# SyncE loads the next expert's first weights ahead of its x and the third unit later; GpSimd places two pooled steps between the last sums of v

## What is computed

```python
out_d = sm_attn(q_d, k_d, v_d)            # q_d, k_d, v_d: means over 4 positions (144 of 576)
out_up = np.repeat(out_d, factor, axis=2)
mask = np.abs(pos[:, None] - pos[None, :]) < factor
scores = np.where(mask, scale * np.matmul(q, k.transpose(0, 1, 3, 2)), -1000000000.0)
...
x = out_up + np.matmul(attn, v)
...
expert_idx = np.argmax(x @ w_gate, axis=1)
h = np.maximum(np.einsum('ecd,edf->ecf', disp, w1), 0.0)   # disp: the tokens of each expert
y = np.einsum('ecf,efd->ecd', h, w2)
...
h = x @ w_in
g = h * np.tanh(np.log1p(np.exp(h)))
return g @ w_out
```

## Time and profile before

| | before |
|---|---|
| median of 3 runs | 476.28 us (473.52 to 480.75) |
| the profiled execution | 477.65 us, span of its trace 475.5 us |
| TensorE busy | 447.9 us, 94% of the span |
| VectorE, ScalarE, GpSimd busy | 280.7, 230.1, 137.2 us |
| share of TensorE in the chain that ended last | 84% |
| moved by DMA | 74.97 MB, mean 158 GB/s |

### The profile page before, as it was taken

One profiled execution on the slowest core, in us unless ns is written; L12 is line 12 of the kernel. 1 busy time (PEld: TensorE's weight loads), 2 busy tenths in 40 slices (PEclk: granted clock), 3 DMA queues, 4 the chain that ended last, 5 costly groups with the idle time before them and its releaser, 6 DMA issues.

```text
span 475.5 us, 10038 instructions
## 1 busy us (share of the span) xinstructions
PE 447.9 (94%) x3380; PEld 412.8 (87%) x3381; DVE 280.7 (59%) x665; ACT 230.1 (48%) x631; POOL 137.2 (29%) x136
## 2 busy tenths in 40 slices
PE   8869898989879999999999999999999999999993
PEld 7658687878879999999999898899988999988982
DVE  7879577679202102102111599888888888888873
ACT  2756665642313323332223566655665655656541
POOL 9587325111000000000004455433253333433202
PEclk9979899599989999999999999999999999999998
DMA  9999999232867988996846234123141121321001
GB/s 186 196 193 152 166 379 347 101 112 74 293 240 243 357 300 281 350 311 207 281 159 207 82 88 45 43 88 90 44 143 57 49 83 45 90 110 44 1 0 66
DMA packets 72143, 74.97 MB, mean 158 GB/s; under 512 B 32816, under 2 KB 47920, under 8 KB 72112
## 3 DMA queue, kind: packets, MB, share of 16 engines
q1 hardware_dynamic: 70384, 69.84, 51.0%
q0 software_dynamic: 1728, 4.72, 2.6%
HBM read 65.11 MB, written 9.44 MB: 157 GB/s over the span
## 4 chain that ended last, share of the span: by engine, by line
PE 84%; DVE 6%; ACT 4%; issue 3%; DMA 1%; SPq 1%; POOLq 0%; POOL 0%; ACTq 0%; DVEq 0%
PE ps L1174 79%; ACT pr L703 2%; PE ps L1256 2%; PE ps L1421 1%; DMA qk_tok<-in_q 1%; PE ps L1302 1%; SPq L431 1%; DVE mx L928 1%; DVE sme L935 1%; PE ps L1251 0%; DVE qT L901 0%; ACT prT L686 0%; DVE kdT L887 0%; DVE qdT L887 0%; DVE gL L1080 0%
## 5 line engine op out<-in xcount | busy, mean ns | idle before, releaser
L637 POOL TENSOR_TENSOR wiL<-raw,wiH 128x512 fp32r<-128x512 f32 x48 | 62.5, 1303 | 251.5 <-ACT wiH L686 148.3
L1174 PE MATMUL ps<-xe,raw 128*128 128x128 f32 (+2 forms) x512 | 71.7, 302 | 4.7 <-issue 3.9
L1174 PEld LDWEIGHTS ps<-xe,raw 128*128 128x128 f32 x512 | 70.4, 194 | 5.6 <-issue 4.4
L1174 PE MATMUL ps<-hid,raw 128*128 128x128 f32 (+2 forms) x512 | 70.8, 297 | 0.0
L1174 PEld LDWEIGHTS ps<-hid,raw 128*128 128x128 f32 x512 | 69.0, 191 | 0.0
L1174 PE MATMUL ps<-x2H,wiH 128*128 128x384 f32 x192 | 65.1, 339 | 0.3 <-DVE x2L L1080 0.3
L1174 PE MATMUL ps<-x2L,wiH 128*128 128x384 f32 x192 | 65.3, 340 | 0.0
L1174 PE MATMUL ps<-x2H,wiL 128*128 128x384 f32 x192 | 64.6, 337 | 0.0
L1174 PE MATMUL ps<-woH,gH 128*128 (+1 forms) x144 | 56.9, 395 | 2.5 <-DVE gL L1080 2.5
L1174 PE MATMUL ps<-woH,gL 128*128 (+1 forms) x144 | 57.2, 397 | 0.0
L1174 PE MATMUL ps<-woL,gH 128*128 (+1 forms) x144 | 56.7, 394 | 0.0
(11 more groups left out here) (140 smaller groups left out, 769.1 us busy)
## 6 DMA issues: line engine op xcount, KB each, us to landing
raw<-in_moe_w SPq DMA_DIRECT2D x32, 1024.0 KB
raw<-in_moe_w_in SPq DMA_DIRECT2D x24, 512.0 KB
x_by_expert<-x_sb SPq DMA_DIRECT2D x1, 4608.0 KB, 15.5
xg<-x_by_expert SPq DMA_DIRECT2D x8, 512.0 KB, 3.6
wo_in<-in_moe_w_out SPq DMA_DIRECT2D x8, 512.0 KB
v<-in_v SPq DMA_DIRECT2D x4, 576.0 KB
qk_tok<-in_k SPq DMA_DIRECT2D x8, 256.0 KB, 4.8
qk_tok<-in_q SPq DMA_DIRECT2D x8, 256.0 KB, 5.1
```

The source lines that it names most:

```text
L637: nc.gpsimd.tensor_tensor(wiL[:, r, :, :], raw_wi_tile(r), wiH[:, r, :, :].bitcast(F32), ALU.subtract).then_inc(s_wil, 1)
L1174: return T.matmul(out_, a, b, start=start, stop=stop, skip_group_check=True)
```

## The change

In SyncE's program the x of expert e is now issued in the body of expert e, behind unit 0 and ahead of unit 1; the load of expert 1's x ahead of the loop is gone; unit 2 waits for `s_y`, the end of `result` of the expert before, in place of `s_w2u`; and the loop now runs over all seven experts. In GpSimd's program the placing of the first two pooled steps stands between sum j = 2 and sum j = 3.

```diff
             sp.wait_ge(s_xg, 16)
-            sp.wait_ge(s_xet, K1)
-            sp.wait_ge(s_xt3, 1)
-            load_x(1)
-
-            def expert(e, last):
+
+            def expert(e):
 
                 sp.wait_ge(s_h, e * M1 - M1 // 2)
                 load_unit(e, 0)
+                sp.wait_ge(s_xet, e * K1)
+                sp.wait_ge(s_xt3, e)
+                load_x(e)
                 sp.wait_ge(s_h, e * M1)
                 load_unit(e, 1)
-                sp.wait_ge(s_w2u, e)
+                sp.wait_ge(s_y, e * M2)
                 load_unit(e, 2)
-                if not last:
-                    sp.wait_ge(s_xet, (e + 1) * K1)
-                    sp.wait_ge(s_xt3, e + 1)
-                    load_x(e + 1)
                 sp.wait_ge(s_h, e * M1 + 1)
                 load_unit(e, 3)
                 load_wo(e)
...
-            for j in range(KH, B * KH):
-                sum_v(j)
+            sum_v(KH)
+            pool.wait_ge(s_vd, KH + 1)
+            place_od(FIRST_DOWN[0])
+            place_od(FIRST_DOWN[0] + 1)
+            sum_v(KH + 1)
             pool.wait_ge(s_vd, B * KH)
-            for n in range(NS):
+            for n in range(FIRST_DOWN[0] + 2, NS):
                 if is_down(n):
                     place_od(n)
```

More of the change, by code:

```diff
@@ L529, in expert @@
                 load_wo(e)
-            with sp.Fori(1, E - 1) as e:
-                expert(e, False)
-            expert(E - 1, True)
+            with sp.Fori(1, E) as e:
+                expert(e)
             wi_v = w_in.rearrange("(k p) f -> p k f", p=P)
```

## The result

| | before | changed |
|---|---|---|
| median (4 runs each) | 475.1 us (473.52 to 480.75) | 488.49 us (487.59 to 489.44) |
| ratio to before | 1 | 1.0293, interval 1.0247 to 1.034 |
| the profiled execution | 477.65 us, span 475.5 us | 489.44 us, span 487.3 us |
| TensorE busy | 447.9 us, 94% | 451.1 us, 93% |

The changed kernel is 2.9% slower; the forecast of 489.4 us lies 0.9 us above its median. But the parts of the sum came out otherwise than forecast, as the trace shows.

A forecast was written before the change was run, and what follows sets the result against it. TensorE, busy 94% of the span, was taken as the bound, so late loads cost time. Waits 9.8 + clock 3.3 + rest 0 = 13.1 us on the 476.28 us median gave 489.4 us, range 481.5 to 495 us.

The forecast's parts named there:

- The x: Expert stage: TensorE waits for the next expert's x, 9.8 us in all, ends 6.6 and 13.3.
- The model: SyncE's load queue: 2.25 us fixed plus bytes at 389 GB/s, up to 1.7 us later; T is an expert's start.
- Expert 0: Transposes of expert 1's x, loaded behind unit 0: a wait of 0.9 to 2.5 us, taken as 1.7.
- Expert 1: Transposes of the next x in expert 1: no wait, since unit 2 leads by 3.6 us.
- The stall and its clock: Ahead of and in expert 1: the 3.63 us stall and 1.67 us of slow clock stay, 0 in the sum.
- the stall is code loading, and it eases: Rival, ahead of expert 1: stall halved, its clock drop gone, 3.5 us back, 486 us; chance 0.12.
- The clock: Behind the two 3.5 us waits TensorE's clock falls to 0.50: 3.3 us, ends nothing and 5.0.
- The rest: Other loads in time, taken as 0; GpSimd's part 0, ends 0.6 us won and 1.0 lost.
- one of its signs: TensorE idle for x in experts 0, 2, 3, 4, none in 1, 5, 6; the 3.63 us stall still there.
- not slower, the stall was unit 0: Rival, start of expert 1: earlier unit 0 removes stall and slow clock, -5.3 us, 471.0 us; chance 0.04.

The follow-up runs named there:

- u2_late: The kernel before with one edit, unit 2 waiting for the end of `result` (`s_y`): 473.76 us, ratio 1.0035.
- x_behind: The kernel before with each x behind unit 0 and the loop over all seven experts, unit 2 and GpSimd as before: 479.97 us, ratio 1.0196.
- pool_only: The kernel before with GpSimd's part of the change alone: 472.7 us, ratio 1.0013.

## Why the prediction held

**The x.** Right in mechanism and near in size. The forecast had waits of 1.7, 0, 3.5, 1.1 and 3.5 us for experts 0 to 4; measured are 2.50, 1.59, 3.81, 0.83 and 3.56. The model put the landing at T + 13.4 to T + 15.1. By the timeline the transposes came at T + 14.7 and 14.4 at 128 columns, and T + 14.1 at 160, so the middle was near, and the error of 1.7 us read from one row was right to be counted in. By the fit of the Trainium skill (DMA: Bandwidth & Descriptors, Anatomy of one DMA — SWDGE (gpsimd) path), made for another path, the estimate was a landing at T + 12.0 and waits of 1.3 us at 128 columns; measured are 3.8 and 3.6.

**Expert 0** was a little too small: 2.50 us is the far end of the term (0.9 to 2.5), and it brought a slow clock of its own, which only the upper end of the clock term allowed for.

**Expert 1** is the first term that failed. It was put at no wait because "its T stands behind the stall of 3.63 us, in which the held-back unit 2 already moves". The stall went, the lead with it, and the wait was 1.59 us: its transposes came at T + 14.9, as late as behind a full train. (The rival below, that the stall eases, should have brought this term with it.)

**The stall and its clock** is the second. The sum left both as they were; 3.63 + 1.67 = 5.3 us came back, and with them the 0.24 us ahead of expert 5. The rival "the stall is code loading, and it eases" was nearest in mechanism, at a chance of 0.12 and for two thirds of the size (3.5 us). Its stated cause, the queue being less loaded, was wrong: u2_late has the emptier queue and the whole stall, x_behind the loaded one and no stall. What fits the runs is that the wait for the x in expert 0 gave the code time to arrive: the four kernels with such a wait have a stall of 0.28 us or none.

**The clock.** 3.3 us forecast for two stretches. There were three new ones: from the transposes to the next expert, 6.28 - 4.59 = 1.69 us in expert 2 and 6.30 - (4.84 - 0.24) = 1.70 us in expert 4, where the stretch before still held the stall of 0.24 us, and in expert 0 3.63 - 1.89 = 1.74. Together 5.1.

**Why the sum was still right:** waits 12.3 instead of 9.8, clock 5.1 instead of 3.3, the stalls and their clock -5.5 instead of 0. That is 11.9, and 12.5 by the starts in the timelines (at four of the five waits the transposes began 0.16 us or so later than the wait alone makes them), against 13.1. Misses of +4.3 and -5.5 us cancel. The waits, the larger part of the sum, were understood; that the total came out this near was luck.

**The rest** held, but for one of its signs: a fifth wait, for expert 1's turn, and no stall of 3.63 us. Unit 2, unit 3 and the dense layer's first loads were in time (no wait of TensorE for `raw` in the stage; 61.3 us from expert 5 to the dense layer in both). The sum j = 3 of v ran from 50.17 us, VectorE's small operation at 45.24 took 0.15 us, and the expert stage began at 113.07 us, within the 1 us allowed. GpSimd's part is worth nothing that the runs can tell. The rival "not slower, the stall was unit 0" is refuted as a forecast, since the x came late. Its cause falls by u2_late, where the queue had all but run empty, with unit 0 landed, 1.7 us before the stall ended.

## What to carry to other kernels

Where one queue carries all loads, ask of each load how many bytes stand ahead of it when it is issued and how much time its user leaves it; an edit that costs next to nothing alone, as u2_late, can cost where another has used up the same slack. Put a small, early-needed transfer ahead of a large, later-needed one. And a stall that belongs to nobody ("issue") may be code loading at the first turn of a long loop: a wait just ahead can hide it, as here, so a forecast should ask whether it may keep both.

## What was not expected of the hardware

- The start of expert 1 came 4.3 to 4.7 us behind the start of one load of 16 KB of code in the five kernels with a stall of 1 us or more, with the data queue at 336 GB/s or at 49. One of four code paths less took 2.05 us off a stall of 3.63.
- Beside GpSimd's sum a small operation of VectorE lost more, for its size, than a large one: `sme` on 128x4 numbers took 0.15 us alone and 0.94 us beside a sum (pool_only), `pr` on 128x560 numbers 0.96 us at 50.28 us, where no sum ran, and 1.52 us beside one.
- The attention stage, the same code in all but GpSimd's few steps, ended and the expert stage began between 108.15 us (u2_late) and 113.80 us (before) from one profiled execution to the next. That may be part of why the medians of the same kernel before lay between 470.77 and 475.1 us; only one trace of it was kept. It is why the lengths of the expert stage, not the totals, carry the smaller readings here; where neither the waits nor the stall changed (before and pool_only) they agree within 0.23 us.
